# Attention and expert kernel on one Trainium2 core: gate logits of a group of tiles in 32-column strips

## What is computed

```
scores = (q @ k^T) / sqrt(64)                        # batch 4, 8 heads, 576 positions, head size 64
ret    = (scores * decay[h]) @ v                     # decay[h] = gamma_h ** (i - j) for j <= i, else 0
x      = ret, heads side by side                     # 2304 x 512
noisy  = x @ w_gate + log1p(exp(x @ w_noise)) * noise  # 8 experts
top-2 of noisy per token, softmax of the two as weights
x      = sum over the two experts of weight * relu(x @ w1[e]) @ w2[e]      # 512 -> 1024 -> 512
h      = x @ w_in                                    # 512 -> 2048
out    = (h * cos(h)) @ w_out
```

## Time and profile before

| | us |
|---|---|
| median of 3 runs | 943.97 (942.25 to 944.18) |
| the profiled execution | 940.39 |
| its span, first to last instruction | 938.6 |
| TensorE busy | 927.2 (99%) |
| VectorE busy | 562.8 (60%) |
| ScalarE busy | 482.3 (51%) |
| GpSimd busy | 95.8 (10%) |
| mean granted TensorE clock | 0.998 of full |

### The profile page before, as it was taken

One profiled execution on the slowest core, in us unless ns is written; L12 is line 12 of the kernel. 1 busy time (PEld: TensorE's weight loads), 2 busy tenths in 40 slices (PEclk: granted clock), 3 DMA queues, 4 the chain that ended last, 5 costly groups with the idle time before them and its releaser, 6 DMA issues.

```text
span 938.6 us, 16655 instructions
## 1 busy us (share of the span) xinstructions
PE 927.2 (99%) x5978; PEld 831.0 (89%) x5978; DVE 562.8 (60%) x1124; ACT 482.3 (51%) x853; POOL 95.8 (10%) x93
## 2 busy tenths in 40 slices
PE   8999999999999999999999999999999999999998
PEld 7889888888989888898988889999889898998987
DVE  4788745565555556443332155667787767877665
ACT  2556627654646465453532155555555655655444
POOL 2266610000000000000000223001100100000000
PEclk9999999999999999999999999999999999999999
DMA  9988667889999999985327259887667755666551
GB/s 362 333 326 287 210 165 244 199 293 291 330 305 318 310 329 268 279 244 169 96 67 278 80 178 324 307 307 258 230 244 268 278 206 212 247 246 241 201 232 57
DMA packets 113112, 230.43 MB, mean 246 GB/s; under 512 B 47384, under 2 KB 71640, under 8 KB 104856
## 3 DMA queue, kind: packets, MB, share of 16 engines
q1 hardware_dynamic: 107288, 210.73, 67.4%
q0 software_dynamic: 5760, 18.88, 5.6%
HBM read 157.65 MB, written 61.70 MB: 234 GB/s over the span
## 4 chain that ended last, share of the span: by engine, by line
PE 93%; DMA 2%; issue 1%; ACT 1%; POOL 1%; DVE 1%; SPq 0%; POOLq 0%; ACTq 0%
PE ps L1950 21%; PE ps L1780 18%; PE ps L1762 18%; PE ps L1936 16%; PE ps L1912 4%; PE ps L1877 3%; PE ps L1865 3%; PE ps L1686 2%; PE ps L1709 2%; PE ps L1701 2%; PE ps L1734 2%; PE ps L1800 1%; PE ps L1814 1%; DMA qk<-qk 1%; PE ps L1852 1%
## 5 line engine op out<-in xcount | busy, mean ns | idle before, releaser
L1950 PE MATMUL ps<-w_sb,g_hi 128*128 128x512 f32 x576 | 180.3, 394 | 0.0
L1762 PE MATMUL ps<-xs,w_hi 128*128 (+1 forms) x784 | 173.2, 303 | 0.0
L1762 PEld LDWEIGHTS ps<-xs,w_hi 128*128 128x128 f32 x784 | 131.2, 188 | 3.1 <-issue 0.2
L1373 DVE TENSOR_TENSOR w_lo<-raw,w_hi 128x1024 fp32r<-128x1024 f32 x48 | 58.8, 1225 | 123.0 <-ACT w_hi L878 123.0
L1762 PE MATMUL ps<-xs,w_lo 128*128 (+1 forms) x392 | 118.7, 303 | 0.0
L1936 PE MATMUL ps<-x_odd,w_sb 128*128 128x320 f32 x672 | 116.9, 309 | 0.0
L1936 PEld LDWEIGHTS ps<-x_odd,w_sb 128*128 128x128 f32 x672 | 107.0, 188 | 9.4 <-DVE h_sb L1530 0.3
L1950 PE MATMUL ps<-w_sb,g_lo 128*128 128x512 f32 x288 | 112.4, 390 | 0.0
L878 ACT ACTIVATE w_hi<-raw 128x1024 fp32r<-128x1024 f32 x48 | 50.9, 1060 | 117.2 <-PE ps L1780 117.2
L1950 PEld LDWEIGHTS ps<-w_sb,g_hi 128*128 128x128 f32 x576 | 101.1, 188 | 9.5
L1780 PE MATMUL ps<-w_hi,hs_lo 128*128 128x512 f32 (+1 forms) x245 | 96.8, 395 | 0.0
(11 more groups left out here) (199 smaller groups left out, 1554.6 us busy)
## 6 DMA issues: line engine op xcount, KB each, us to landing
w_sb<-w_pairs SPq DMA_DIRECT2D x24, 1792.0 KB, 8.1
w_sb<-w_pairs SPq DMA_DIRECT2D x40, 1024.0 KB, 9.5
raw<-weights SPq DMA_DIRECT2D x64, 512.0 KB, 4.8
w_pairs<-stage SPq DMA_DIRECT2D x24, 1024.0 KB, 7.5
qk<-qk SPq DMA_DIRECT2D x18, 512.0 KB, 6.8
kv<-kv SPq DMA_DIRECT2D x18, 512.0 KB, 5.4
y_slots<-zeros_sb SPq DMA_DIRECT2D x33, 256.0 KB
raw_pair<-pairs SPq DMA_DIRECT2D x8, 1024.0 KB, 8.8
```

The costliest lines, as they stand in the source:

```text
L1373: tt(w_lo[:, at], raw[:, f % 2, :], w_hi[:, at].bitcast(F32), ALU.subtract).then_inc(split_done, 1)
L1762: last_one = nc.tensor.matmul(ps[5 + half][:, 0:HALF], w[:, at:at + P], xs[:, bass.ds(g % 2, 1), a, k, half * HALF:(half + 1) * HALF].rear ...
L1950: last_one = nc.tensor.matmul(ps[j][:, :], a[:, slot % 2, part, j * C:(j + 1) * C], w2_sb[slot % 3][:, hl, part * DM:(part + 1) * DM], sta ...
```

## The change

The logits of a tile are no longer computed in its own step. When the last tile of a group has been reached, TensorE computes them for all of the group's tiles (`gate_strips`): the stationary operand is now `wg`, padded with zeros from 16 to 32 columns, and the moving one is `xT`, 128 columns; tile i of the group writes partitions 32i to 32i+31 of the group's bank, and the loop goes over the tiles inside and over the feature blocks outside. ScalarE copies the result (up to 128 x 128) to `gateT`, and TensorE transposes it back in one go (`turn_gates`), after the row transposes of that step. `xT` has four buffers instead of two. The softplus waits for the group's transpose, GpSimd ahead of tile 12 for that of the last group.

```diff
@@ constants, buffers, semaphores
+PARTS = 256
+STRIP = P // GMAX
+XT_BUFS = 4
...
-            xT = [keep(f"xT{i}", [P, KD_TILES, C], F32, st) for i in range(2)]
-            wg = keep("wg", [P, KD_TILES, 2 * E], F32, st)
+            xT = [keep(f"xT{i}", [P, KD_TILES, C], F32, st) for i in range(XT_BUFS)]
+            wg = keep("wg", [P, KD_TILES, STRIP], F32, st)
+            gateT = keep("gateT", [P, C], F32, st)
...
+        strips_done, strips_copied = sem("strips_done"), sem("strips_copied")
@@ gpsimd, scatters of the last tiles
                 elif t == LATE_FROM + 3:
-                    pool.wait_ge(logit_done, NT)
+                    pool.wait_ge(logit_done, NG)
@@ scalar, softplus(k); vector, first_choice(k)
-                act.wait_ge(logit_done, hi)
+                act.wait_ge(logit_done, k + 1)
...
-                z = logit_bank(k)[0:C, 0:n * 2 * E].rearrange("c (t e) -> c t e", e=2 * E)[:, :, E:2 * E]
+                z = logit_bank(k)[0:C, 0:n * STRIP].rearrange("c (t e) -> c t e", e=STRIP)[:, :, E:2 * E]
...
-                both = logit_bank(k)[0:C, 0:n * 2 * E].rearrange("c (t e) -> c t e", e=2 * E)
+                both = logit_bank(k)[0:C, 0:n * STRIP].rearrange("c (t e) -> c t e", e=STRIP)
@@ scalar, step(s), behind the softplus
+                t = s - 2
+                if t + 1 in GROUPS[1:]:
+                    k = group_of(t)
+                    n = GROUPS[k + 1] - GROUPS[k]
+                    act.wait_ge(strips_done, k + 1)
+                    nc.scalar.activation(gateT[0:n * STRIP, :], logit_bank(k)[0:n * STRIP, PARTS:PARTS + C], ACT.Copy
+                                         ).then_inc(strips_copied, 1)
                 t = s - 1
                 if 0 <= t < NT:
                     act.wait_ge(out_done, t + 1)
-                    above(act, logit_done, t - 1)
-                    above(act, rows_ps_done, t - 1)
-                    nc.scalar.activation(xT[t % 2][:, :, :], ps[O_BANK[t % 2]][:, :].rearrange("p (k c) -> p k c", k=KD_TILES),
+                    if t >= XT_BUFS:
+                        act.wait_ge(strips_done, group_of(t - XT_BUFS) + 1)
+                        act.wait_ge(rows_ps_done, t - XT_BUFS + 1)
+                    nc.scalar.activation(xT[t % XT_BUFS][:, :, :], ps[O_BANK[t % 2]][:, :].rearrange("p (k c) -> p k c", k=KD_TILES),
                                          ACT.Copy).then_inc(xT_done, 1)
@@ tensor
+            def gate_strips(k_):
+                lo, hi = GROUPS[k_], GROUPS[k_ + 1]
+                above(pe, ranked, k_ - 1)
+                for k in range(KD_TILES):
+                    for i in range(hi - lo):
+                        last_one = nc.tensor.matmul(logit_bank(k_)[i * STRIP:(i + 1) * STRIP, PARTS:PARTS + C], wg[:, k, :],
+                                                    xT[(lo + i) % XT_BUFS][:, k, :], start=k == 0, stop=k == KD_TILES - 1,
+                                                    skip_group_check=True)
+                last_one.then_inc(strips_done, 1)
+
+            def turn_gates(k_):
+                n = (GROUPS[k_ + 1] - GROUPS[k_]) * STRIP
+                pe.wait_ge(strips_copied, k_ + 1)
+                nc.tensor.transpose(logit_bank(k_)[0:C, 0:n], gateT[0:n, :], ident[0:n, 0:n]).then_inc(logit_done, 1)
@@ tensor, step(s), tile t = s - 2
-                    k_ = group_of(t)
...
-                    if t == GROUPS[k_]:
-                        above(pe, ranked, k_ - 1)
                     pe.wait_ge(xT_done, t + 1)
-                    at = (t - GROUPS[k_]) * 2 * E
-                    for k in range(KD_TILES):
-                        last_one = nc.tensor.matmul(logit_bank(k_)[0:C, at:at + 2 * E], xT[t % 2][:, k, :], wg[:, k, :],
-                                                    start=k == 0, stop=k == KD_TILES - 1)
-                    last_one.then_inc(logit_done, 1)
+                    if t + 1 in GROUPS[1:]:
+                        gate_strips(group_of(t))
                     above(pe, x_done, t)
                     for k in range(KD_TILES):
-                        last_one = nc.tensor.transpose(ps[5][0:C, k * P:(k + 1) * P], xT[t % 2][:, k, :], ident)
+                        last_one = nc.tensor.transpose(ps[5][0:C, k * P:(k + 1) * P], xT[t % XT_BUFS][:, k, :], ident)
                     last_one.then_inc(rows_ps_done, 1)
+                    if t + 1 in GROUPS[1:]:
+                        turn_gates(group_of(t))
```

More of the change, by code:

```diff
@@ L206, in build @@
             ret = [keep(f"ret{i}", [C, 2, PAIRS, C], F32, st) for i in range(3)]
-            xT = [keep(f"xT{i}", [P, KD_TILES, C], F32, st) for i in range(2)]
-            wg = keep("wg", [P, KD_TILES, 2 * E], F32, st)
-            used = -(-ATTN_W // 8) * 8 + 3 * 2 * DM + 3 * 2 * DM + 2 * DM + 2 * DM + DM // 2 + 3 * 2 * DM + 2 * DM + KD_TILES * 2 * E
+            xT = [keep(f"xT{i}", [P, KD_TILES, C], F32, st) for i in range(XT_BUFS)]
+            wg = keep("wg", [P, KD_TILES, STRIP], F32, st)
+            gateT = keep("gateT", [P, C], F32, st)
+            used = -(-ATTN_W // 8) * 8 + 3 * 2 * DM + 3 * 2 * DM + 2 * DM + 2 * DM + DM // 2 + 3 * 2 * DM + XT_BUFS * DM + KD_TILES * STRIP + C
             keep("below_rows", [P, 2 * RING * CHUNK + TPU * DM - used], F32, st)
@@ L2006 @@
     gates = np.concatenate([moe_w_gate, moe_w_noise], axis=1).reshape(KD_TILES, P, 2 * E).transpose(1, 0, 2)
+    gates = np.pad(gates, ((0, 0), (0, 0), (0, STRIP - 2 * E)))
     arrays = {
```

## The result

The change ran in 937.09 us (median of 4 runs, 936.58 to 937.51), the kernel before beside it in 943.53. The recorded ratio is 0.9956, with a 95% interval of 0.9937 to 0.9975: faster by 0.4%, beyond the 0.2% that a measurement can tell. It is not the quotient of the two medians, which is 0.9932 and lies just outside that interval; how it is weighed is not known here. The forecast was 937.1 with 934.3 to 942.2.

The account below looks back on a forecast made before the run. TensorE was taken to bound the kernel (93% of the chain), with VectorE and ScalarE late next. Gains of 2.9 by step 6 and 4.1 in the middle, none at the hand-over, 6.9 in all: 943.97 - 6.9 = 937.1, range 934.3 to 942.2.

Parts of the forecast that it names:

- Strips: Batched logits on TensorE: 32 ns a record, 1.02 us for a group of four tiles, 0.77 for three.
- (a): Strips on TensorE overlap only two by two: 64 ns a record, gain 3.3 us, 940.7; chance 0.14.
- (b): Strips on TensorE do not overlap: 124 ns a record, 5.7 us slower, 949.7; chance 0.10.
- Step 6: Start of attention step 6, after TensorE-bound early steps: at 29.35 instead of 32.25, 2.9 us gained.
- 3 x 0.99: Steps 2, 3 and 4 each lose their logits on TensorE, 0.99 us apiece, 2.97 gained.
- rival (c): DMA loads bind the early steps until 32 us, so their 2.9 goes: gain 4.0, 939.9; chance 0.12.
- Middle: Steps 6 to 16: 52.7 us instead of 56.8, 4.1 gained of the 7.4 that TensorE frees, VectorE limiting.
- the walk: Step-by-step layout of the attention part from row durations: step 13 at 61.85, step 17 at 82.06.
- Hand-over: Stretch before the first expert product: ScalarE's chain sets it, nothing more gained; product at 93.85, 6.9 gained in all.
- Rival (e): At the hand-over, gathered planes or GpSimd's scatters don't come 6.9 earlier: gain about 2, 942; chance 0.07.
- over 1 us: At the hand-over, VectorE uses the gathered planes at 95.47, over 1 us before ScalarE gets to them at 96.7.
- rival (d): Clock fall around the first expert products: avoided 935.1, or once more 939.1; sum keeps one fall; chance within forecast's 0.57.

Follow-up runs that it names:

- edit (1): Changed kernel with the scaling of k in tiles 7, 11, 12 and 15 moved from VectorE to ScalarE: 934.9 us (0.9934), once more 935.66 us (0.9953).

## Why the prediction was right, and where it was not

**Strips.** The term of the sum held: 1.02 forecast, 1.01 and 1.05 measured, for four. Three take as long as four (1.01, not 0.77). Copy and turn-back: `gateT` 0.28 (0.30 forecast), TensorE's loss behind it 0.1 to 0.2 (0.15). Rivals (a) and (b) fell with the prices (with neighbours of four, 31.5 and neither 64 nor 124), though (b)'s premise, that a lone record takes what the column count says, was also the forecast's own ("one alone would be near 128 ns"). The right price came from a wrong scale: two strips in turn cost 46 and not the 64 of the values.

**Step 6: 2.5 for 2.9.** Mis-sized term: "3 x 0.99". The transposes behind lost their 0.11, so 3 x 0.88. The loads, rival (c), grazed only: step 5 began 0.16 later than that pace, and its first weight load, at 24.34, waited 0.30 for qk. It is the third and shortest of these waits (us in all, times, longest):

```profile
PEld ps L1714 <- DMA qk<-qk: 3.6, 3, 1.8
```

That is one of the forecast's own signs of being wrong ("if TensorE waits for qk or kv behind step 2"), and it cost 0.16. Step 5 took 5.34 for 5.24. The earlier step 2 (11.64 against 11.86) offsets most of the two.

**Middle: 1.6 for 4.1. This is the step that failed.** "Every step is laid out from row durations" took mean or lone durations for VectorE, as if the neighbours on GpSimd moved along with it. They don't: GpSimd goes by the end of TensorE's values (`above(pool, out_done, t - 1)`), and VectorE, once late against TensorE, meets the scaling of q at other operations. Start by start against the walk: steps 6 to 10 took 23.2 (23.4 forecast), steps 11 and 12 together 11.2 (9.1; the noise sum 1.25 in the first, the running sums 1.99 and the wait of 1.3 in the second), steps 13 to 16 20.8 (20.2). Steps 11 and 12 hold 2.1 of the missing 2.5. That the collision costs this is shown for step 12 by taking it away (1.4 back); for step 11 it is read from the timeline only. The 52.58 of the edit (1) agrees with the walk, but partly for another reason: it takes four scalings off VectorE as well. So how much of the 2.5 is collision and how much VectorE's plain load is not shown beyond the 1.4. The clean test, the scaling of q on another engine than GpSimd, wasn't tried; leaving it out would change the choice of experts, and with it which rows are scattered.

**Hand-over: -0.8 for 0.** Rival (e), given 0.07, is partly what happened. The chain that ended last runs through GpSimd and the DMAs here:

```profile
79.53 1.27 POOL x_slots L742
80.80 0.30 issue
81.10 5.64 DMA x_slots<-x_sb,pos_x
86.75 0.02 issue
86.76 4.87 DMA planes<-x_slots
```

The gather began at 86.76 where it had begun at 89.90: 3.1 earlier, not 6.9. The chain ahead of it, up to 80.80, is GpSimd's: scalings of q and scatters one behind the other, with hardly a wait between them. It begins with a scatter that waited for VectorE's positions, with the change and before:

```profile
66.96 1.01 POOL L742 DMA_INDIRECT x_slots<-x_sb,pos_x  x1 [4.22 <-DVE pos_x L1240]
```

```profile
69.48 1.01 POOL L737 DMA_INDIRECT x_slots<-x_sb,pos_x  x1 [2.60 <-DVE pos_x L1227]
```

So 2.5 of the 3.1 were there at its start. The walk had step 13 at 61.85 and it started at 64.12; the positions fall in that step, and so 2.3 of the 3.8 that are missing here (an estimate from these two starts) are the lateness of steps 11 and 12 over again. From the positions to the last scatter of tile 7 GpSimd then took 14.1 instead of 15.4, and that scatter 5.64 instead of 5.0 until the gather began. With VectorE relieved by edit (1) the positions' scatter starts at 63.76. An engine that was 55% busy in the middle (31.13 of 56.80) has no slack left behind the positions. The margin of "over 1 us" between VectorE's and ScalarE's use of the gathered rows was the margin of a kernel in which they came early. VectorE's second choice starts behind that gather (its first use at 91.72 waited 0.39), and the count behind the sums, and so TensorE's 1.6.

**The clock**, rival (d): one fall stayed, as the sum had it, in the profiled execution (granted clock, as a share of full speed, 0.65 from 96 to 98 and 0.50 to 100, the lower level, 1.2 GHz, after a hand-over in which TensorE waited 2.5 of 12.6). But it isn't there in each execution: the second ones of both kernels hold 1.00 from 88 to 108. The second one of the kernel before fell at other places, from 6 to 12 and from 132 to 138 us (0.50 in the middle 2 us of each), and the second of the change nowhere by more than a trace (mean clock 0.9996). That is part of why the expert part scattered. Over the 85 runs of the kernel before in the later measurements, those with a mean clock of 0.998 took 940.3 us on average, those with 0.996 941.5, those with 0.994 943.4. It is scatter on both sides, and no term of the change is seen in it.

**Sum.** 2.5 + 1.6 - 0.8 + 0.1 = 3.4 between the two profiled executions, whose own times differ by 940.39 - 937.02 = 3.4. Against the forecast of 6.9: 0.4, 2.5 and 0.8 short. The second executions give 2.4 + 2.6 - 1.1 + 3.1 = 7.0, of which 3.1 lie behind the first product, where the change has no term. The time came out right because the reference lay 2.1 to 3.7 above the four later medians, 2.9 above the one beside which the change was measured again. The direction and the mechanism of the strips were right; the size of the gain was not, and its agreement in the total is luck.

## What to carry to other kernels

When a change frees the bounding engine, the others don't move along in step. Lay out not only their busy time but who runs beside whom: a VectorE operation with both inputs in SBUF can last until a GpSimd scaling ends, here 1.2 us more for an operation of 0.17. Shifting one such operation here only moved the collision; taking work off VectorE, onto ScalarE, shortened the middle by 2.6 us in the first execution and by 1.8 in the second, and a gain in the whole time is likely.

A forecast in absolute time is as good as its reference: with three runs the median was 2.9 off, and that is some 40% of the effect forecast. A forecast of the difference, and of the profiled execution, would have shown the miss at once.

## What the runs showed of the hardware

- A f32 record with 32 weight columns and 128 moving ones: 75 ns in one strip, 46 with two strips in turn, 42 with three, 31.5 with four. The last is close to the 29 of the state updates, as if some 30 ns were what a record costs at least here; that wasn't tested.
- Four transposes of 128 columns take 0.59 behind 64-column state updates, 0.48 behind the logits and 0.49 behind the strips. Why is open.
- Back-to-back pieces on GpSimd keep VectorE out as one long operation does (1.65 beside 1.69), and cost more in all (1.69 to 2.15 for 1.27).
- In a collision it is VectorE that was stretched, even where its record starts first (80.74, GpSimd's at 81.24), while GpSimd's scaling stays at 1.26 to 1.30. In that case a scatter ran on GpSimd until 81.22; whether it already held VectorE isn't shown (running sums beside a scatter, at 60.78, kept their 0.17). Operations with one input in PSUM (`ret`, `state`) were not stretched beside any scaling in the traces of the two kernels.
- TensorE stopped for 0.2 to 1.3 us within a group of matmuls in some executions, with nothing in the profile that releases it: 1.28 within the scores of step 17 in one version, 0.60 in step 15 in another, 0.36 in step 12 of the kernel before. What these are is open.
- The granted clock fell to 1.2 GHz for 3 to 6 us at a place that changes from one execution to the next: 100 to 106 us in one of the kernel before, 6 to 12 and 132 to 138 in another, 62 to 70 in two edits of the change, whose TensorE had waited 1.3 for the running sums just before, as it had in the change's own two executions, where no fall followed there.
